# Weight halves moved out of the third large tile, and the last second layer set between the first period's products, in a Strassen MLP chain on one core

## The reference

```python
# attention: 4 batches, 8 heads, 768 positions, head 64; chunks of 32 queries see 8 memory keys
# and a window of 56 keys around them; out is the softmax-weighted sum of the values
x = attn_out.transpose(0, 2, 1, 3).reshape(3072, 512)
h = maximum(maximum(x @ w1, x @ w2), x @ w3)        # w1, w2, w3: 512 x 768
y = h @ w_out1                                      # 768 x 512
h = y @ w_in2                                       # 512 x 2048
g = where(h >= 1, h, where(h <= -1, 0, (h + 1) ** 2 / 4))
out = g @ w_out2                                    # 2048 x 512
```

## Time and profile before

| what | value |
|---|---|
| runs (3) | 970.91, 972.83, 973.87 us; median 972.83 |
| the profiled execution | 973.86 us, of which 972.1 us are the span of its instructions |
| granted TensorE clock | 1.0 of full speed |
| PE busy | 946.4 us, 97% of the span |
| DVE, ACT, POOL busy | 485.1, 434.8, 453.0 us |

### The profile page before, as it was taken

How to read it: one execution, slowest core, us unless ns; L and a number is a source line. 1 busy time by engine, 2 the same in 40 slices (tenths; PEclk the granted TensorE clock), 3 DMA queues, 4 the chain that set the end, 5 groups by cost and what they waited for, 6 DMA issues and landing times.

```text
span 972.1 us, 19065 instructions
## 1 busy us (share of the span) xinstructions
PE 946.4 (97%) x7806; PEld 876.8 (90%) x7806; DVE 485.1 (50%) x755; ACT 434.8 (45%) x713; POOL 453.0 (47%) x628
## 2 busy tenths in 40 slices
PE   6999999999999999899899999999999999999998
PEld 5999999999989999899799889989889888989897
DVE  4673576667466775862353533445333544333231
ACT  3342343443343443332464645636365554545354
POOL 2669985878188825630223333232323343332321
PEclk9999999999999999999999999999999999999999
DMA  9777899999499948993344546444454434554331
GB/s 371 253 285 248 310 328 367 394 385 392 155 375 386 329 172 286 307 354 140 121 174 152 176 152 236 147 178 175 169 206 155 174 121 171 162 196 171 126 115 65
DMA packets 50328, 223.01 MB, mean 229 GB/s; under 512 B 5953, under 2 KB 10049, under 8 KB 42689
## 3 DMA queue, kind: packets, MB, share of 16 engines
q0 software_dynamic: 31936, 165.17, 47.4%
q1 hardware_dynamic: 18304, 56.63, 16.3%
HBM read 178.00 MB, written 43.78 MB: 228 GB/s over the span
## 4 chain that ended last, share of the span: by engine, by line
PE 50%; issue 0%; ACT 0%; DVE 0%; ACTq 0%
PE mlp_ps L622 9%; PE mlp_ps L623 9%; PE mlp_ps L621 9%; PE attn_ps L623 3%; PE scores_ps L623 3%; PE attn_ps L622 3%; PE scores_ps L622 3%; PE scores_ps L621 3%; PE attn_ps L621 3%; PE trans_ps L623 2%; PE trans_ps L622 2%; PE trans_ps L621 1%; ACT ramp L1153 0%; ACT out_stage L904 0%; DVE up_m L1485 0%
## 5 line engine op out<-in xcount | busy, mean ns | idle before, releaser
L904 ACT ACTIVATE up_m<-mlp_ps 128x384 f32<-128x384 f32 x293 | 143.3, 489 | 315.1 <-PE mlp_ps L623 288.4
L621 PE MATMUL mlp_ps<-yc,wa 128*128 128x384 f32 x472 | 160.8, 341 | 10.1 <-ACT up_m L904 6.9
L622 PE MATMUL mlp_ps<-yc,wa 128*128 128x384 f32 x472 | 158.4, 336 | 0.0
L623 PE MATMUL mlp_ps<-yc,wa 128*128 128x384 f32 x472 | 158.0, 335 | 0.0
L508 POOL DMA_DIRECT2D wa<-wa_scratch x59 | 31.8, 540 | 229.2 <-PE mlp_ps L623 223.8
L621 PE MATMUL mlp_ps<-yc,wb 128*128 128x384 f32 x354 | 119.4, 337 | 1.0 <-DMA wb<-wb_scratch 1.0
L528 POOL CAST wo<-wo_raw 128x1024 fp32r<-128x1024 f32 x32 | 33.3, 1040 | 186.8 <-PE trans_ps L623 186.8
L622 PE MATMUL mlp_ps<-yc,wb 128*128 128x384 f32 x354 | 119.0, 336 | 0.0
L623 PE MATMUL mlp_ps<-yc,wb 128*128 128x384 f32 x354 | 118.4, 335 | 0.0
L1491 DVE SCALAR_TENSOR_TENSOR ramp<-ramp,up_m 128x768 f32<-128x768 f32 x64 | 62.5, 976 | 111.7 <-ACT ramp L1153 111.7
L621 PEld LDWEIGHTS mlp_ps<-yc,wa 128*128 128x128 f32 x472 | 88.6, 188 | 19.4 <-ACT up_m L904 9.6
(11 more groups left out here) (172 smaller groups left out, 2146.2 us busy)
## 6 DMA issues: line engine op xcount, KB each, us to landing
wa<-wa_scratch POOLq DMA_DIRECT2D x59, 1024.0 KB, 5.3
wb<-wb_scratch POOLq DMA_DIRECT2D x59, 768.0 KB, 7.2
qk_raw<-qk_l SPq DMA_DIRECT2D x24, 768.0 KB, 7.9
wo_raw<-w_out POOLq DMA_DIRECT2D x32, 512.0 KB, 4.0
wa_scratch<-stage_a POOLq DMA_DIRECT2D x30, 512.0 KB, 5.4
v_raw<-v_l SPq DMA_DIRECT2D x24, 512.0 KB, 7.4
wb_scratch<-stage_a POOLq DMA_DIRECT2D x30, 384.0 KB, 6.7
y_scratch<-up_m SPq DMA_DIRECT2D x32, 192.0 KB, 1.9
```

The lines of the kernel that those rows point to most:

```text
L621: pe.matmul(out_ap, a_hi, b_hi, start=first, stop=False, skip_group_check=beside)
L622: pe.matmul(out_ap, a_lo, b_hi, start=False, stop=False, skip_group_check=beside)
L623: return pe.matmul(out_ap, a_hi, b_lo, start=False, stop=last, skip_group_check=beside)
L904: return act.activation(o, i, ACT.Copy)
```

## The change

It takes the weight halves out of the third large tile, and out of the periods 6, 12 and 15. One half (12) is made in the second layer of the second small tile, three (21 to 23) in that of the first large tile and three (31 to 33) in that of the second; there `split_begin` and `split_end` follow one another at once. After half 12 POOL waits until all eight low parts of the first large tile's operands are made. The staging buffers alternate for all halves, and `yc_high` of the first y tile waits for all 34 stores.

In the last second layer, the eight sums stand between products 2 to 6 of the second MLP's first period, after `L2_FOLLOWS`; only the first four blocks of sums 0 to 2 stand ahead of product 2. ACT's list follows that order (`first_period`). Two new buffers take the waits away that the order would bring: `y_last` holds all eight sums for their stores, `ramp_first` the first period's ramp. `split_wo(1)` also waits for `g_split` of 2, the last `g_low` of period 0. Some waits of ACT go elsewhere (`yc_high` of the second y tile waits for the stores of y and for `g_split`, in place of the last first-layer product).

```diff
+L2_FOLLOWS = {0: (), 2: (0,), 3: (1,), 4: (2, 3), 5: (4, 5, 6), 6: (7,)}
-EARLY, AHEAD, LAST_PAIR, HALVES = 4, 12, 30, 2 * ITEMS
-HALF_IN = {g: AHEAD + g for g in range(HALVES - AHEAD)}
+EARLY, AHEAD, HALVES = 4, 12, 2 * ITEMS
+L2_HALVES = (1, 3, 3)
+PAIRS_WITH_HALF = [g for g in range(2 * PAIRS_S) if g not in (6, PAIRS_S + 3, PAIRS_S + 6)]
+HALF_IN = {g: AHEAD + sum(L2_HALVES[:g // PAIRS_S + 1]) + i for i, g in enumerate(PAIRS_WITH_HALF)}
...
-            start = (1 if n >= LAST_PAIR else n % 2) * (W_SUMS // 2 + W_COLS)
+            start = n % 2 * (W_SUMS // 2 + W_COLS)
...
             def split_wo(g):
                 if g == 1:
                     pool.wait_ge(l2_done, 2 * KD * TILES_S)
+                    pool.wait_ge(g_split, 2)
...
+            def halves_in_layer2(n, window):
+
+                for i in range(L2_HALVES[window]):
+                    split_begin(n + i)
+                    split_end(n + i)
...
+            halves_in_layer2(AHEAD, 0)
+            pool.wait_ge(x_split, 8)
             for g in range(PERIODS_S):
...
                 load_wb(g + 2)
+                if g % PAIRS_S == PAIRS_S - 1 and g + PAIRS_S < PERIODS_S:
+                    halves_in_layer2(HALF_IN[g] + 1, g // PAIRS_S + 1)
...
-            layer2_large(TILES_S - 1)
+            l2_first_blocks(TILES_S - 1)
             for i in range(2, 7):
                 product(0, i)
+                for x in L2_FOLLOWS[i]:
+                    l2_product(TILES_S - 1, x)
...
             def y_part(v, x):
                 b = x % 4
                 act.wait_ge(l2_done, 2 * KD * v + x + 1)
-                act.wait_ge(y_stored[b], 16 * (TILES + 2 * v + x // 4))
-                if x < 4:
-                    act.wait_ge(h2_lo_done, 4 * KFP * (v + 1))
-                copy(y_stage[:, b], l2_bank(v, x)).then_inc(y_copied, 1)
+                if v < TILES_S - 1:
+                    act.wait_ge(y_stored[b], 16 * (TILES + 2 * v + x // 4))
+                    if x < 4:
+                        act.wait_ge(h2_lo_done, 4 * KFP * (v + 1))
+                copy(y_slot(v, x), l2_bank(v, x)).then_inc(y_copied, 1)
...
                 elif v == 1:
-                    act.wait_ge(l1_done, 7 * PERIODS_S)
+                    for y in y_stored:
+                        act.wait_ge(y, 16 * 2 * TILES_B)
+                    act.wait_ge(g_split, 2)
                 else:
                     for w in w_stored:
-                        act.wait_ge(w, 16 * LAST_PAIR)
+                        act.wait_ge(w, 16 * HALVES)
...
+            def first_period():
+
+                for i in (0, 2, 3, 4):
+                    copy_product(0, i)
+                    for x in L2_FOLLOWS[i]:
+                        y_part(TILES_S - 1, x)
+                bent(0, 0)
+                squared(0, 0)
+                for x in L2_FOLLOWS[5]:
+                    y_part(TILES_S - 1, x)
+                copy_product(0, 6)
+                bent(0, 1)
+                squared(0, 1)
+                for x in L2_FOLLOWS[6]:
+                    y_part(TILES_S - 1, x)
+
+            first_period()
+            for g in range(1, PERIODS):
                 u, p = divmod(g, PAIRS)
-                if g:
+                if g > 1:
                     copy_product(g - 1, 6)
                     bent(g - 1, 1)
                 copy_product(g, 0)
-                if g == 0:
-                    for x in range(2 * KD):
-                        y_part(TILES_S - 1, x)
-                if g:
+                if g > 1:
                     squared(g - 1, 1)
-                    g_high(g - 1, 0)
-                    g_high(g - 1, 1)
+                g_high(g - 1, 0)
+                g_high(g - 1, 1)
```

More of the change, by code:

```diff
@@ L52 @@
 L2_AHEAD = 3
+L2_FOLLOWS = {0: (), 2: (0,), 3: (1,), 4: (2, 3), 5: (4, 5, 6), 6: (7,)}
 ITEMS = PAIRS_S + PAIRS
-EARLY, AHEAD, LAST_PAIR, HALVES = 4, 12, 30, 2 * ITEMS
-HALF_IN = {g: AHEAD + g for g in range(HALVES - AHEAD)}
-WO_LOAD, WO_SPLIT = HALVES - AHEAD + 1, HALVES - AHEAD + 3
+EARLY, AHEAD, HALVES = 4, 12, 2 * ITEMS
+L2_HALVES = (1, 3, 3)
+PAIRS_WITH_HALF = [g for g in range(2 * PAIRS_S) if g not in (6, PAIRS_S + 3, PAIRS_S + 6)]
+HALF_IN = {g: AHEAD + sum(L2_HALVES[:g // PAIRS_S + 1]) + i for i, g in enumerate(PAIRS_WITH_HALF)}
+WO_LOAD, WO_SPLIT = PERIODS_S - 4, PERIODS_S - 2
 WA_COLS, WB_COLS = 4 * 2 * P, 3 * 2 * P
@@ L146, in build_attention_and_two_mlps @@
         out_stage = sbuf(ctx, "out_stage", [SUBS, DM])
+        sbuf(ctx, "h2_end", [GPT * (QK + HALF_HEADS * CPG * D) + 3 * H * WIN + HALF_HEADS * P + P + 8 * TT + A_STAGES * A_COLS + W_RAW
+                             + 2 * KF1 * DM + 4 * KF1 * TT - 8 * TT - Y_SUMS - 4 * Y_COLS - 10 * DM - 10 * TU - SUBS * DM])
+        y_last = sbuf(ctx, "y_last", [2 * KD, TT])
+        ramp_first = sbuf(ctx, "ramp_first", [2, TU])
         x_hi, x_lo = (x0_hi, x1_hi), (x0_lo, x1_lo)
@@ L164, in staged_last @@
                 return None
-            return n - 1 if n < EARLY or n >= LAST_PAIR else n - 2
+            return n - 1 if n < EARLY else n - 2
         def w_operand(n, op, j):
@@ L180, in build_attention_and_two_mlps, with ramp_of, y_slot @@
                    scores_ps[:, BANK:2 * BANK], trans_ps[:, :])
+        def ramp_of(g):
+            return ramp_first[:, :, :] if g == 0 else ramp[:, :, :]
+        def y_slot(v, x):
+            if v < TILES_S - 1:
+                return y_stage[:, x % 4]
+            return y_last[:, x]
         def scores_of(n):
@@ L377, in store_part @@
                 tokens = slice(TU * (v + 1) + TT * t, TU * (v + 1) + TT * (t + 1))
-                sp.dma_start(y_scratch[:, d, tokens], y_stage[:, b]).then_inc(y_stored[b], 16)
+                sp.dma_start(y_scratch[:, d, tokens], y_slot(v, x)).then_inc(y_stored[b], 16)
             def load_groups(groups):
@@ L771, in l2_blocks, with l2_first_blocks, l2_product, layer2_large @@
                     last.then_inc(l2_done, 1)
-            def layer2_large(v):
+            def l2_first_blocks(v):
                 for x in range(L2_AHEAD):
                     l2_blocks(v, x, range(KF1 - 2))
-                for x in range(L2_AHEAD):
-                    l2_blocks(v, x, range(KF1 - 2, KF1))
-                for x in range(L2_AHEAD, 2 * KD):
-                    l2_blocks(v, x, range(KF1))
+            def l2_product(v, x):
+                l2_blocks(v, x, range(KF1 - 2 if x < L2_AHEAD else 0, KF1))
+            def layer2_large(v):
+                l2_first_blocks(v)
+                for x in range(2 * KD):
+                    l2_product(v, x)
             def strassen_tile(v):
@@ L1132, in copy_product @@
                     if g == 1:
-                        for y in y_stored:
-                            act.wait_ge(y, 16 * 2 * TILES_B)
+                        act.wait_ge(h2_lo_done, 4 * KFP * TILES_S)
                     if g >= 2:
@@ L1145, in bent @@
                     act.wait_ge(g_split, 2 * (g - 1) + f + 1)
-                else:
-                    act.wait_ge(l2_done, 2 * KD * TILES_S)
-                act.activation(ramp[:, f], up[:, g % 2, f].rearrange("p t c -> p (t c)"), ACT.Relu, bias=half_col[:, 0:1],
+                act.activation(ramp_of(g)[:, f], up[:, g % 2, f].rearrange("p t c -> p (t c)"), ACT.Relu, bias=half_col[:, 0:1],
                                scale=0.5).then_inc(ramp_done, 1)
@@ L1152, in squared @@
                 act.wait_ge(ramp_done, 2 * g + f + 1)
-                act.activation(ramp[:, f], ramp[:, f], ACT.Square).then_inc(square_done, 1)
+                act.activation(ramp_of(g)[:, f], ramp_of(g)[:, f], ACT.Square).then_inc(square_done, 1)
             def g_high(g, f):
@@ L1159, in g_high @@
                     act.wait_ge(down_done, SUBS * (g - 1))
-                copy(g_hl[:, g % 2, 0, f], ramp[:, f]).then_inc(g_hi_done, 1)
+                copy(g_hl[:, g % 2, 0, f], ramp_of(g)[:, f]).then_inc(g_hi_done, 1)
             def copy_out(u, s):
@@ L1166, in copy_out @@
                 copy(out_stage[:, s], out_acc[s]).then_inc(out_copied, 1)
-            for g in range(PERIODS):
+            def first_period():
[14 more added lines that the diff above has]
+            for g in range(1, PERIODS):
                 u, p = divmod(g, PAIRS)
-                if g:
+                if g > 1:
                     copy_product(g - 1, 6)
@@ L1490, in g_values @@
                 dve.wait_ge(folded, 3 * (g + 1))
-                dve.scalar_tensor_tensor(ramp[:, f], ramp[:, f], 1.0, up[:, g % 2, f].rearrange("p t c -> p (t c)"),
+                dve.scalar_tensor_tensor(ramp_of(g)[:, f], ramp_of(g)[:, f], 1.0, up[:, g % 2, f].rearrange("p t c -> p (t c)"),
                                          ALU.min, ALU.max).then_inc(g_done, 1)
@@ L1495, in g_low @@
                 dve.wait_ge(g_hi_done, 2 * g + f + 1)
-                dve.tensor_tensor(g_hl[:, g % 2, 1, f], ramp[:, f], g_hl[:, g % 2, 0, f].bitcast(F32),
```

(1 more changed line is left out.)

## The result

The kernel with the change takes 961.06 us (median of 6 runs, 960.32 to 962.52); the kernel before, in 6 runs beside it, 973.45 (970.91 to 976.59). The ratio is 0.9861, with a 95% interval of 0.9843 to 0.9879. The profiled execution took 960.89 us, its span is 959.1; that of before was 972.1. So 13.0 us went by the spans and 12.4 by the medians, where 10.6 were forecast.

A forecast was written before the change was run, and what follows sets the result against it. PE, busy 97% of the span, was taken as the bound, so only its late starts could be won back. From 973.86 us: -6.6 - 2.4 - 3.4 + 1.8 = -10.6, so 963.3 us (median perhaps 962.3), range 960.0 to 967.5.

The forecast's parts named there:

- the second layers: Windows that take the moved halves: a loss of 1.8 us together, bounds 0 and 6.0.
- the first two tiles: First two large tiles: milder collisions and skipped halves in periods 6, 12 and 15 gain 2.4 us.
- Third tile: Third large tile: 7.2 us lost there, 0.6 left in periods 2 and 5, so a gain of 6.6 us.
- Rival 4: Third tile's stalls are DVE's own yc work, not POOL's, so no gain there: 969.9 us, chance 0.05.
- the small tile's half: One `split_end` in the second small tile delays DVE's sums and product 1: 0.9 us lost, bounds 0 and 1.0.
- the collisions of periods 8 and 15: First two large tiles: DVE pairs slowed beside POOL; both go, gaining 1.0 and 0.9 us.
- a stall of ACT in period 12: Period 12 without a half eases one more of five waits, put at 0.5 us.
- First period: Second MLP, period 1's product 0 to first `down`: 4.1 us lost, 0.7 left, gain 3.4, bounds 0 and 4.1.
- A `split_end`: Price to DVE in the second layers: 2.4 us if caught ahead of both subtractions, otherwise 1.5.
- the copy of sum 3: Second large tile's second layer, ACT: 4.7 us of work ahead against 3.8 slack, so 0.9 lost, bounds 0 and 2.5.
- Rival 1: Second layers cost their upper bounds, ACT's `y_part` being held in both large ones: 967.5 us, chance 0.17.
- rival 2: Interleaved first period wins nothing, as ACT still has `g_high` to do in period 1: 966.7 us, chance 0.10.

The follow-up runs named there:

- h: Changed kernel with half 12 taken out of the small tile, halves of periods 0 to 5 one period later, and one again in period 6: 963.67 us.
- b: Kernel before with only the new order of the last second layer and first period, halves placed as of old: 971.07 us, ratio 0.9971.
- c: Changed kernel without the wait of `split_wo(1)` for `g_split`, so it goes once the last sum is done: 962.39 us.
- d: Changed kernel with the arithmetic of the seven second-layer halves cut to 8 columns, all waits and transfers kept: 960.81 us.
- i: Kernel before with the third large tile's loads of made weights issued by SP instead of POOL, halves whole: 970.57 us in one run.
- e: Kernel before with the arithmetic of the third tile's four halves cut to 8 columns, DMAs and waits kept: 975.40 us, ratio 1.0001.
- f: Changed kernel with both subtractions of each half run twice in the two large second layers: 970.96 us.
- j: Kernel before with both the third tile's half arithmetic cut to 8 columns and its loads of made weights issued by SP: 968.09 us in one run.

## Where the prediction failed, and where it held

**What failed.** The forecast of 10.6 us fell short of the 13.0 measured because two of its terms were mis-sized: the second layers, put at a loss of 1.8 us, lost 0.4, and the first two tiles, put at a gain of 2.4, gained 3.4. Both errors go the same way, so no luck hid them. In the bottom of the range there is also a slip: 960.8 less a us is 959.8, not 960.0. The 959.3 of the ratio lies below either.

**Third tile: right in sum, half right in cause.** 6.6 forecast, 6.48 measured, and the residue stood where it was put, 0.19 and 0.1 in periods 2 and 5. I had named blocked pairs, store waits and late loads together, and led with the pair of 3.37 us. The factors are 2.0 for POOL's arithmetic and 4.7 for having the loads in POOL's queue, of which 2.6 are stalls behind blocked pairs all the same. The sum did not depend on this division, since all of it left the tile. Rival 4 (DVE's own load) fell: with all the operand work for y in place, only the 0.6 us of periods 2 and 5 are left.

**First two tiles: the step that failed second.** 2.4 forecast, 3.2 measured, or 3.4 without the 0.19 that the small tile's half costs. The forecast counted the collisions of periods 8 and 15, and both went. It also put 0.5 on a stall of ACT in period 12, and that stall stayed, 0.36 us of idle PE before and after. It read the wait of `load_wa` in period 6 only as what delays the next subtraction, and put nothing on the loads: that they then come late for PE was in the waits of before as 0.6 us for a `load_wb`, which the earlier trace rows do not hold. With its restart that is 0.7 us of the gain; in h, where it is back, PE waits 2.4 us for the `load_wa` itself.

**First period: right.** 3.4 forecast, 3.60 measured; b shows it by itself and c shows that 1.1 of it hangs on the wait for `g_split`. The interleaving cost nothing: L2 + period 0 is 32.24 us in both orders. Of the 0.7 said to be left, 0.5 was.

**Second layers: the step that failed first.** 1.8 forecast, 0.4 measured by d. The price of a half was too high. A `split_end` was taken at 2.4 us from a pair caught ahead of both subtractions; in the windows the engines took turns and it cost 1.8. So the copy of sum 3, nearest to its limit, was 3.0 later and not 4.7, inside a slack of 3.8, and the 0.9 put there are 0. The small tile's half was put at 0.9 and cost 0.2, and the first large tile, put at 0, cost 0.2. Rival 1 fell with it, rival 2 with the tail.

The sum of what was missed: 1.4 in the second layers, 1.0 in the first two tiles, 0.2 in the first period, less 0.1 in the third tile. To rounding, these are the 2.4 us between 10.6 and 13.0.

## What to carry to other kernels

When an engine both computes and issues the loads of another, read each of its waits twice: for what its own work then collides with, and for the loads queued behind it. The two are tied: here taking the loads out of POOL's queue won 4.7 us in the third tile, 1.5 of them waits for loads and 2.6 collisions that came out milder, against 2.0 for taking away its arithmetic. Work moved into a window costs by where it lands on the copies and operands with the least slack, so price it against that slack, and check how late the moved engine leaves the window. And test such causes in all four corners, since with the arithmetic gone the loads took back half of the 3.9 us of stalls that went with it.

## What the runs showed that I had not expected

- Two engines that take turns both stretch: DVE's pair of sums took 2.94 us instead of 1.15, and POOL's subtractions 1.60 and 1.33 instead of 1.31 and 1.01. DVE lost the full 2.35 us where both of POOL's subtractions went ahead of one of its instructions, 382.29 against 382.51; begun at 383.43 beside a subtraction from 383.50, the pair in i lost 1.1 and POOL 0.6.
- A store and a load through DRAM in a row vary: POOL waited 5.2 us (before), 5.7 (b), 5.8 (h) and 6.0 (e) for the same store, and PE for the `load_wa` behind it not at all in before, 1.3 in b, 2.4 in h and 4.0 in e.
- Around PE's waits of 2.7 us (f) and 4.0 us (e) the granted clock fell to 0.50, for 3.4 and 6.8 us; behind those of 2.4 us (h) and 2.3 us (i) it stayed at 1.00. No run tested the cause by itself.
- With the arithmetic of four halves nearly gone, POOL's waits for its stores more than doubled, 6.6 to 14.2 us, and with loads out of its queue as well they reached 21.2, as j's waits of POOL from 366 to 446 us show:

```profile
POOL stage_a L488 <- DMA wb_scratch<-stage_a: 21.2, 3, 8.0
```
